# Third score tile as block-diagonal whole-array products, and a super-block's max-out work inside its own eight rounds

## The reference

```python
scores = scale * np.matmul(q, k.transpose(0, 1, 3, 2))        # 4 x 8 heads, 576 x 576, head size 64
kth = np.partition(scores, -32, axis=-1)[..., -32:-31]
scores = np.where(scores >= kth, scores, -1000000000.0)
attn = softmax(scores);  x = (attn @ v), heads side by side   # 2304 x 512
h = np.maximum(np.maximum(x @ w1, x @ w2), x @ w3)            # 512 -> 768
x = h @ w_out                                                 # 768 -> 512
logits = x @ w_gate + modality_bias[modality_id]
e_idx = np.argmax(logits, axis=1)                             # one of 8 experts
out[mask] = gate_w * (np.maximum(x[mask] @ w1[e], 0.0) @ w2[e])   # 512 -> 1024 -> 512
```

## Time and profile before

| | |
|---|---|
| time, median of 3 runs | 972.83 us (972.33 to 973.17) |
| the profiled execution's own time | 972.48 us |
| its span in the profile | 970.9 us |
| mean granted TensorE clock | 0.991 of full speed |
| busy: TensorE | 918.1 us (95%) |
| busy: VectorE | 716.7 us (74%) |
| busy: GpSimd, ScalarE | 657.4 us (68%), 580.5 us (60%) |

### The profile page before, as it was taken

The page is one execution under the profiler, slowest core; times in us unless marked ns, Lnnn a source line. Parts: engine busy times, 40 slices in busy tenths (PEclk is TensorE's granted clock), DMA queues, the critical chain, the costliest instruction groups (busy, mean ns, idle before and its releaser), DMA issues.

```text
span 970.9 us, 18073 instructions
## 1 busy us (share of the span) xinstructions
PE 918.1 (95%) x5324; PEld 680.9 (70%) x5325; DVE 716.7 (74%) x2191; ACT 580.5 (60%) x1226; POOL 657.4 (68%) x623
## 2 busy tenths in 40 slices
PE   4698788999999999999999999999989999999997
PEld 1255667677676677676686677685865988998996
DVE  5999999999999999999999999995304431151211
ACT  2577777778687787787787787775314221252221
POOL 7999988988888897988888887965252222222221
PEclk9999998999999999999999999999999999999999
DMA  6722211312121122121212121111051053106110
GB/s 207 242 58 57 58 46 43 117 46 70 52 58 57 48 64 67 57 58 53 69 47 68 42 69 57 42 36 36 12 189 44 14 194 98 43 33 227 54 54 32
DMA packets 61591, 70.85 MB, mean 73 GB/s; under 512 B 7776, under 2 KB 42880, under 8 KB 61504
## 3 DMA queue, kind: packets, MB, share of 16 engines
q1 hardware_dynamic: 57584, 59.43, 20.1%
q0 software_dynamic: 3920, 10.40, 3.4%
HBM read 59.05 MB, written 10.76 MB: 72 GB/s over the span
## 4 chain that ended last, share of the span: by engine, by line
PE 83%; issue 6%; DVE 5%; ACT 1%; POOL 1%; another core or an unknown queue 0%; DVEq 0%; POOLq 0%
PE m_ps L1378 18%; PE m_ps L1455 10%; PE m_ps L1399 10%; PE s_ps L1321 9%; PE t_ps L1335 8%; PE s_ps L1438 8%; PE o_ps L1351 7%; PE m_ps L1392 6%; DVE top L1124 3%; PE o_ps L1438 3%; PE m_ps L1406 2%; DVE upper L1126 1%; PE t_ps L1427 1%; DVE work L1126 1%; PE m_ps L1403 1%
## 5 line engine op out<-in xcount | busy, mean ns | idle before, releaser
L777 POOL TENSOR_TENSOR scores<-scores,below 128x576 f32<-128x576 f32 x144 | 200.3, 1414 | 69.9 <-ACT below L909 69.2
L1378 PE MATMUL m_ps<-xT,w_sb 128*128 128x192 f32 x1152 | 203.5, 333 | 1.2 <-ACT xT L953 1.2
L1378 PEld LDWEIGHTS m_ps<-xT,w_sb 128*128 128x128 f32 x1152 | 190.9, 194 | 2.2 <-ACT xT L953 1.5
L1124 DVE MAX8 top<-upper 128x8 f32<-128x288 f32 x384 | 159.4, 448 | 0.4 <-issue 0.3
L1126 DVE MATCH_REPLACE8 upper<-top,upper 128x288 f32<-128x288 f32 x288 | 125.3, 443 | 0.2 <-issue 0.2
L917 ACT ACTIVATE probs<-scores,shift 128x576 f32<-128x576 f32 x144 | 111.4, 783 | 15.0 <-issue 15.0
L1335 PEld LDWEIGHTS t_ps<-ident,probs 128*128 128x128 f32 x720 | 80.9, 142 | 55.6 <-issue 49.7
L946 ACT COPY probsT<-t_ps 128x640 f32<-128x640 f32 x192 | 103.2, 563 | 25.3 <-PE t_ps L1335 21.8
L785 POOL TENSOR_SCALAR probs<-probs,inverse 128x576 f32<-128x576 f32 x144 | 105.3, 752 | 15.0 <-DVE inverse L1108 15.0
L1335 PE MATMUL t_ps<-ident,probs 128*128 128x128 f32 x720 | 108.9, 283 | 6.2 <-ACT probsT L946 6.1
L1321 PE MATMUL s_ps<-k_sb,q_sb 64*64 64x288 f32 (+1 forms) x576 | 100.1, 454 | 15.4 <-ACT fall L934 6.1
(11 more groups left out here) (203 smaller groups left out, 1719.7 us busy)
## 6 DMA issues: line engine op xcount, KB each, us to landing
k_sb<-keys_t SPq DMA_DIRECT2D x48, 288.0 KB, 3.0
v_sb<-values SPq DMA_DIRECT2D x48, 256.0 KB, 2.7
raw<-e_w SPq DMA_DIRECT2D x12, 1024.0 KB
q_sb<-queries_t SPq DMA_DIRECT2D x48, 96.0 KB, 1.9
maxout_rows<-x_rows SPq DMA_DIRECT2D x18, 256.0 KB, 2.0
w_sb<-w SPq DMA_DIRECT2D x2, 1536.0 KB, 10.5
v_sb<-values SPq DMA_DIRECT2D x48, 32.0 KB, 2.6
stage<-w_t SPq DMA_DIRECT2D x1, 1536.0 KB, 8.9
```

The lines of the kernel that those rows point to most:

```text
L777: nc.gpsimd.tensor_tensor(scores[:, r % RING, i, :], scores[:, r % RING, i, :], below[:, i, :], ALU.subtract).then_inc(masked_ready, 1)
L1124: nc.vector.max(best, src).then_inc(topk_step, 1)
L1378: ins = nc.tensor.matmul(dst[:, a * BLK:(a + 1) * BLK], w_sb[:, w, c, (first + a) * P:(first + a + 1) * P], xT[:, m % 2, c, b % SPAN * BLK ...
```

## The change

Three things are changed together.

1. Tile 2 of the scores becomes two products of the whole array. `q_rest` is a tile of 128 x 128 that holds head 0's last 64 rows in its upper left quarter, head 1's in its lower right, and zeros elsewhere. GpSimd zeroes it once; two small DMAs a round fill the two quarters, beside one for the 128 rows of `q_sb`, so that a round's loads are four DMAs in place of two.
2. `PARTS` and `LAST_PARTS` are written anew. Output tiles 1 and 2 of a super-block, which stood in the eight rounds of the next one, now stand in its own last two rounds; only T and L of those two tiles stay behind.
3. At the end of attention the count comes one round earlier, the dispatch list is written ahead of GpSimd's wait for the last V, VectorE chooses experts ahead of the last round's sums, and two of the first expert's four weight pieces are split inside the first chunk's hidden products.

```diff
-PARTS = [[(0, A[0]), (0, A[1]), (1, ("Y", 1))],
-         [(1, ("X", 1)), (0, A[2])],
-         [(1, ("T", 1)), (0, A[3]), (1, ("L", 1)), (0, A[4])],
-         [(1, ("Y", 2)), (1, ("X", 2))],
-         [(0, A[5]), (0, A[6]), (0, A[7])],
-         [(1, ("T", 2)), (0, A[8]), (1, ("L", 2)), (0, A[9])],
-         [(0, ("Y", 0)), (0, ("X", 0))],
-         [(0, ("T", 0)), (0, A[10]), (0, ("L", 0)), (0, A[11])]]
-LAST_PARTS = PARTS[:1] + [
-    [(1, ("X", 1)), (1, ("Y", 2)), (0, A[2])],
-    [(1, ("X", 2)), (1, ("T", 1)), (0, A[3]), (1, ("L", 1)), (1, ("T", 2)), (0, A[4]), (1, ("L", 2))],
-    [(0, A[5])],
-    [(0, A[6]), (0, A[7])],
-    [(0, ("Y", 0)), (0, ("X", 0)), (0, A[8]), (0, ("T", 0)), (0, A[9]), (0, ("L", 0)), (0, A[10]), (0, A[11])],
+PARTS = [[(0, A[0]), (0, A[1]), (0, A[2])],
+         [(0, A[3]), (0, A[4]), (0, A[5])],
+         [(1, ("T", 1)), (1, ("L", 1)), (1, ("T", 2)), (1, ("L", 2)), (0, ("Y", 0))],
+         [(0, ("X", 0)), (0, ("T", 0)), (0, ("L", 0))],
+         [(0, A[6]), (0, A[7]), (0, A[8])],
+         [(0, A[9]), (0, A[10]), (0, A[11])],
+         [(0, ("Y", 1)), (0, ("Y", 2))],
+         [(0, ("X", 1)), (0, ("X", 2))]]
+LAST_PARTS = [
+    [(0, A[0]), (1, ("T", 1)), (0, A[1]), (1, ("L", 1)), (0, A[2])],
+    [(0, A[3]), (1, ("T", 2)), (0, A[4]), (1, ("L", 2)), (0, A[5])],
+    [(0, ("Y", 0))]] + PARTS[3:6] + [
     [(0, ("Y", 1)), (0, ("Y", 2)), (0, ("X", 1)), (0, ("X", 2))],
     [(0, ("T", 1)), (0, ("L", 1)), (0, ("T", 2)), (0, ("L", 2))]]
...
-COUNT_AT = LAST_START + RPB - 1
-LOAD_AT = COUNT_AT + 1
+COUNT_AT = LAST_START + RPB - 2
+LOAD_AT = COUNT_AT + 2
...
-TURN_AT = {("X", 1): (0,), ("T", 1): (1,), ("T", 2): (2,)}
+TURN_AT = {("T", 1): (0,), ("L", 1): (1,), ("T", 2): (2,)}
...
-                for dst, src, n in ((q_sb, qT, r), (k_sb, kT, k_of)):
-                    sp.dma_start(dst[:, slot, :], src[n, :, :]).then_inc(qk_in[slot], 16)
+                sp.dma_start(k_sb[:, slot, :], kT[k_of, :, :]).then_inc(qk_in[slot], 16)
+                sp.dma_start(q_sb[:, slot, :], qT[r, :, 0:P]).then_inc(qk_in[slot], 16)
+                if r < 2:
+
+                    sp.wait_ge(rest_pads_ready, 1)
+                for h in range(2):
+                    sp.dma_start(q_rest[h * HEAD:(h + 1) * HEAD, slot, h * HEAD:(h + 1) * HEAD],
+                                 qT[r, h * HEAD:(h + 1) * HEAD, P:BLK]).then_inc(qk_in[slot], 16)
...
+            pool.wait_ge(routing_in, 16 * 2)
+            write_list(nc, pool, shared, early, list_dram, range(EARLY))
+
             pool.wait_ge(pv_done, ROUNDS)
             for buf in (info, info2, xg):
                 nc.gpsimd.memset(buf[:, :, :], 0.0).then_inc(cleared, 1)
-            pool.wait_ge(routing_in, 16 * 2)
-            write_list(nc, pool, shared, early, list_dram, range(EARLY))
...
                 if r == RECTIFY_LAST:
-                    for n in range(PIECES):
+                    for n in range(PIECES // 2):
                         steps.append((-1, lambda n=n: high_piece(0, n)))
...
+                if f in FIRST_PIECE_AT:
+                    high_piece(0, FIRST_PIECE_AT[f])
...
             choose_experts(nc, shared, early_part, early, link)
+            full_sums(ROUNDS - 1)
+            inverses(ROUNDS - 1)
             running_counts(nc, dve, early_part, early, link, s_ps[:, 0, :])
...
-                if i < 2:
-
-                    keys = k_sb[:, slot, HALF:SEQ] if i == 0 else k_diff[:, slot, :]
-                    parts = [(h, 0, P, 0, h, keys) for h in range(2)]
-                else:
-                    parts = [(h, P, REST, h * HEAD, half, k_sb[:, slot, half * HALF:(half + 1) * HALF])
-                             for half in range(2) for h in range(2)]
...
+                else:
+
+                    for half in range(2):
+                        ins = nc.tensor.matmul(s_ps[:, half, 0:HALF], q_rest[:, slot, :],
+                                               k_sb[:, slot, half * HALF:(half + 1) * HALF], start=True, stop=True)
```

More of the change, by code:

```diff
@@ L47 @@
 MAX8 = 8
+QK_LOADS = 4 * 16
 CHAIN = 2 * (TOPK // MAX8) - 1
@@ L91 @@
 PIECE = 2 * D * F2 // P // PIECES
+PIECE_AT = {0: 2, 3: 3}
+FIRST_PIECE_AT = {2: 2, 5: 3}
 H_BANKS = 3
-PIECE_AT = {0: 2, 3: 3}
 FIRST_TURNS = ((), (0, 1), ())
@@ L453, in program @@
             xT = hb("xT", [P, 2, DK, SW])
-            q_sb = hb("q_sb", [P, 2, BLK])
+            q_sb = hb("q_sb", [P, 2, P])
+            q_rest = hb("q_rest", [P, 2, P])
             k_sb = hb("k_sb", [P, 2, SEQ])
@@ L707, in _ @@
         def _(pool):
+            nc.gpsimd.memset(q_rest[:, :, :], 0.0).then_inc(rest_pads_ready, 1)
             nc.gpsimd.memset(top[:, :, :, 1:2], HUGE).then_inc(top_pads_ready, 1)
@@ L863, in _ @@
             pool.wait_ge(star_ready, 1)
+            pool.drain()
             for i in range(XT):
@@ L1110, in one_round @@
             def one_round(r):
-                if not in_range(r):
-                    if in_range(r - 1):
-                        full_sums(r - 1)
-                        inverses(r - 1)
-                    return
                 slot, steps = r % FOLD_BUFS, [r * CHAIN_STEPS]
@@ L1169, in _ @@
             dve.wait_ge(sum_pads_ready, 1)
-            for r in range(ROUNDS + 1):
+            for r in range(ROUNDS):
                 one_round(r)
@@ L1210, in h_low_part @@
                     in1=hTh[:, f, :].bitcast(F32), op0=ALU.max, op1=ALU.subtract).then_inc(h_low, 1)
-            for n in range(PIECES):
-                if n == PIECES - 1:
-                    wait_apart(dve, passed, moe_ready, PLACE[SUPERS - 1, ("X", 1)] + 1)
+            for n in range(PIECES // 2):
                 low_piece(0, n)
@@ L1306, in score_tile @@
                 if i == score_order(r)[0]:
-                    pe.wait_ge(qk_in[slot], (r // 2 + 1) * 32)
+                    pe.wait_ge(qk_in[slot], (r // 2 + 1) * QK_LOADS)
                 if scored(r, i) > 1:
                     wait_apart(pe, passed, scores_copied, scored(r, i) - 1)
+                if i == 1:
+                    wait_apart(pe, passed, k_diff_ready, r + 1)
                 if i < 2:
                     keys = k_sb[:, slot, HALF:SEQ] if i == 0 else k_diff[:, slot, :]
-                    parts = [(h, 0, P, 0, h, keys) for h in range(2)]
-                else:
-                    parts = [(h, P, REST, h * HEAD, half, k_sb[:, slot, half * HALF:(half + 1) * HALF])
-                             for half in range(2) for h in range(2)]
-                if i == 1:
-                    wait_apart(pe, passed, k_diff_ready, r + 1)
-                for h, row, rows, part, bank, keys in parts:
-                    ins = nc.tensor.matmul(s_ps[part:part + rows, bank, 0:HALF],
-                                           q_sb[h * HEAD:(h + 1) * HEAD, slot, row:row + rows],
-                                           keys[h * HEAD:(h + 1) * HEAD, :], start=True, stop=True)
+                    for h in range(2):
+                        ins = nc.tensor.matmul(s_ps[:, h, 0:HALF], q_sb[h * HEAD:(h + 1) * HEAD, slot, :],
+                                               keys[h * HEAD:(h + 1) * HEAD, :], start=True, stop=True)
+                else:
+                    for half in range(2):
+                        ins = nc.tensor.matmul(s_ps[:, half, 0:HALF], q_rest[:, slot, :],
+                                               k_sb[:, slot, half * HALF:(half + 1) * HALF], start=True, stop=True)
                 ins.then_inc(scores_ready, 1)
```

8 lines of the change are left out of this document (5 added, 3 removed).

## The result

The changed kernel takes 975.76 us (median of 10, 974.46 to 977.6) and the kernel before 972.67 in the same comparison (972.22 to 976.53): ratio 1.003, 95% interval 1.0018 to 1.0041. It is slower by 0.3%, where the forecast was 955.5 us and a range of 948 to 968. The profiled execution has a span of 974.6 us against 970.9.

What follows compares the result with a forecast made beforehand. TensorE was taken to set the pace from 200 to 640 us, VectorE before that. First expert product 738.0 against 756.1, plus 0.7, gives -17.4: span 953.5, median 955.5 us; range 948 to 968.

Steps and rivals of the forecast that it cites:

- The third tile: Score tile 2 as whole-array products: saves 0.18 us a round where TensorE sets the pace, about 38 rounds, 7 us.
- the estimate that the prediction made from it: Counter-case for the third score tile: if small tiles run independently, the change costs 0.49 us a round, 19 us.
- Rounds 6 to 13: Largest term: early rounds take 17.2 us more work into TensorE's gaps; V of round 14 at 204.0 against 202.4.
- They cost nothing while SyncE waits for scores anyway: Two more 16 KB DMAs a round are free; without that cover, some 0.4 us each on SyncE's queue.
- Each full super-block: Steady state: 110.6 us less 1.5 for the tile plus 2.4 of new stalls, 111.5, four times: +3.6 us.
- X0 to T0: New stall in each super-block: T0 waits for the copy of X0's result, 0.9 us with the semaphores.
- the rival's clause: Rival "Slower", chance 0.05: new waits at T1 to L1 and X0 to T0 lower TensorE's clock on each super-block.
- the rival's own condition: Rival "Slower" (0.05) decides once waits and clock cost over 3.5 us a super-block more than the forecast allows.
- The tail: From V of round 46 to the first expert product: 88.7 us against 112.0 before, 17.2 of it work done earlier.
- T0 now stands before the expert's weights are loaded: Tail: why the 4.22 us wait for T0's copy and the lower clock (7.47 us for 5.20) should go.
- The rival that let a copy be held up for 4 to 7 us in the tail: Rival "New waits are larger", chance 0.22: doubled stalls, +13 us, or expert's weight load holding up a copy; 960 to 969.
- The late weight pieces: Behind the first expert product, two late pieces cost VectorE 2.29 us each; taken as 0.7, bounds 0 and 4.6.

Runs made afterwards that it cites:

- tile_only: Kernel before with only the block-diagonal third score tile and its four loads, schedule and tail as before: 960.77 us, ratio 0.9951.
- mod_later: Changed kernel with the load of the modality ids issued in round 3 of SyncE's list instead of ahead of the rounds: 973.22 us, ratio 1.0019.
- tl_between: Changed kernel with T1, L1, T2, L2 moved from the third round to between the A groups of the first two: 970.70 us, ratio 0.9993.
- before_fives: Kernel before with its 15 list DMAs in fives, each five landed before the next is issued: 964.93 us, ratio 0.9927.
- drains_back: Changed kernel with two removed GpSimd drains restored, in the expert loop and just ahead of it: 970.55 us, ratio 0.9991.
- list_fives: Changed kernel with the 15 list DMAs in fives, all ahead of the wait for the last V, no other edit: 964.43 us, ratio 0.9919.
- after_again: The changed kernel timed once more, unedited, against the kernel before: 974.12 us, ratio 1.0022.

## Why the prediction was wrong

- **The third tile** was right: 0.97 us, 0.19 us per round by its own rows and 0.20 in tile_only, forecast 0.18. The transposes ahead of it and behind it came out at 0.55 and 0.64, not 0.60 and 0.60; only their sum is as forecast. The Trainium skill's TensorEngine Tiling (Array Packing), Tiling Modes, calls the four small tiles independent; by the estimate that the prediction made from it tile_only would have been 0.49 us a round slower, and the runs decide against it here.
- **Rounds 6 to 13** were right in kind: 17.2 us more work were done by V of round 14. The size was off by 2.3 us. The step that failed is "They cost nothing while SyncE waits for scores anyway": at round 3 SyncE doesn't wait, its queue is full of the modality ids, and each load more comes later (mod_later). Of the 2.3 us 2.1 stand already at `kth` of round 2 (54.79 against 52.72 us): 0.4 at the start, for which the prediction allowed 0 to 0.5 and took none, and 1.6 in the round that the issue behind the ids lengthens.
- **Each full super-block** was right in its waits: T to L start to start 1.92 us (0.44 and 1.48), X0 to T0 a wait of 0.75 (0.9 forecast). What was missed is the rival's clause: the clock fell behind the wait of T1's copy in two to four super-blocks of four. The rival had priced a fall at 3.4 us and one at every wait; it was 1.58, and only at the one place. A fall of that size stood in the rows: the clock of 0.88 over 123 to 150 makes 3.2 us lost, of which the fall at 147 accounts for 1.5, and the window 123.10 to 126.50 of the kernel before has 0.50, behind the wait of 3.83 us. With 4.9 us over the forecast in four super-blocks, 1.2 each, the rival's own condition (3.5 each) was not met. But the falls were worth 3 to 6 us, as much as or more than the 3.1 us by which the changed kernel is slower, and so they count towards the sign. The Trainium skill's TensorE: Matmul & The Clock Gate (Part 1) lets idleness throttle; the waits of 1.39 us in tl_between did not do it in any of four places, those of 1.3 us ahead of L did it in some.
- **The tail** holds the step that failed most. It said that the wait of 4.22 us for T0's copy and the lower clock behind it go because "T0 now stands before the expert's weights are loaded". The weights had nothing to do with it: 15 list DMAs in a row made TensorE's increments late, before_fives shows, and the change kept the row and moved it beside the last V, where all engines wait for one increment. It cost 10.7 us in place of 7.4 (8.3 to 10.0 in five other executions with the same row ahead of V). The rival that let a copy be held up for 4 to 7 us in the tail was near in kind, but it too blamed the expert's load. The work itself was counted rightly: 88.65 us without lateness, forecast 88.7, in eight kernels.
- **The late weight pieces** cost 0.72 us (209.65 less 208.93), forecast 0.7 out of bounds of 0 and 4.6. The trace has one wait for them, which the kernel before has not:

```profile
773.85 0.47 PE L1462 MATMUL m_ps<-w2h,hTh 128*128 128x512 f32 x1 [0.63 <-DVE w2l L1202]
```

- **Not counted at all** were the two drains that the change takes out: 3.2 us (drains_back). The list of the change further up doesn't name them either. I had costed what the change adds and moves and had left out what it removes from an engine with time to spare.

Of the forecast's 17.4 us the changed kernel thus gave back 21.1. With T1, L1 and T2 moved, the drains back, q_rest's loads on their own semaphore and the list broken up it takes 954.77 to 954.97 us, and 954.06 with the ids later as well. That this is the forecast's 955.5 us is partly luck: these kernels are 0.6 to 1.6 us behind the forecast to V of round 14 and 1.6 us ahead of it from there to V of round 46.

Without the lateness on either side the change as it stands is worth nothing measurable: 964.43 us (list_fives) against 964.93 (before_fives). Their traces say where the gain goes: 16.0 us are won between V of round 46 and the first expert product, and lost are 3.6 to V of round 14, 8.4 to V of round 46, 0.9 in the expert products and 3.2 behind them.

## What to carry to other kernels

Ask of each wait in a tail which engine's increment was late, and what another engine issued in a row at the time; a load that runs beside it is only a suspect until it is moved. Cost the lines that a change removes as carefully as those that it adds, drains above all. Where a group must wait for a copy of its neighbour's result, put a third group between them, and keep one behind the last transposes of the round, since ScalarE's own chain needs cover too.

## What the runs showed of the hardware

- Indirect DMAs that GpSimd issues one per 1.27 us without a wait between make TensorE's semaphore increments late: by at most 0.7 us with 5 or 6 in a row, by 0.8 and 3.9 us near the end of 9, by 5 us with 10, and by 7.0 to 9.7 us for the latest one with 15 (six traces of the changed schedule). The products themselves are not held. Why, and why one comparison of six was free of it, is open.
- GpSimd's drain at the program's end took 3.49 us where the expert loop holds no drains and 0.29 where it does.
- The load of 2304 ids of 8 bytes held the next issue on SyncE's queue for 3.6 to 6.1 us, against 0.34.
- A wait of 1.3 us on TensorE was followed by 3.4 us at half the clock in some executions and not in others of one kernel (three of four places in the result's trace, two in after_again's). Each such stretch costs 1.6 us.
